# Inverse norm stored ahead of the first tile's load, second weights loaded sooner, ninth mean behind item 3, copies of two means moved

## The chip, the core and the metric

The kernel runs on one core of a Trainium2 chip. A core has five engines, each with a queue of its own: TensorE (PE in the profile; its weight loads are PEld), VectorE (DVE), ScalarE (ACT), GpSimd (POOL) and SyncE (SP, which here only issues DMAs). POOL issues DMAs too: those that add into their target. Both kinds run on the core's 16 DMA engines. Engines wait for each other by semaphores. The metric is the device time of one execution in microseconds (us), lower is better.

## The reference, cut to what matters

```python
X = np.fft.fft(x, axis=1); X = np.fft.fft(X, axis=2)      # x (2, 3008, 256)
x = X.real.reshape(6016, 256)
rms = np.sqrt(np.mean(x * x, axis=-1, keepdims=True) + 1e-06)
xn = x / rms * rms_g
g, val = xn @ w_gate, xn @ w_val                           # 256 -> 1536 each
x = (g / (1.0 + np.exp(-g)) * val) @ w_out                 # 1536 -> 256
h = x @ w_in                                               # 256 -> 2048
out = (h * np.cos(h)) @ w_out2                             # 2048 -> 256
```

## The kernel before, in words

**Stage one, the transform.** The two Fourier transforms are done as matrix products over pairs of tokens that are mirror images (N = 502 pairs make a tile; six tiles, three for each of the two batches). A loop over 34 steps G runs on TensorE: `features(G)`, then `sequence` two or three steps behind. ACT copies two steps' results at a time out of PSUM in `uv_copy(p)`, p = G // 2. The result is u and v, stored to DRAM in pieces (`store_uv`) and loaded again a tile at a time (`load_tile`, `load_u128`).

**The norm.** The rows are cut into nine parts, and each part's mean of squares is numbered 0 to 8 (`MEANS` = 9). For each: ACT squares (`square`, L669), POOL adds the two halves (`add_squares`, L1096), TensorE sums over partitions with one product (`rms`, L504), ACT copies the row out of PSUM adding epsilon (`mean_copy`, L677), and SP spreads it over partitions (`spread_mean`, L334). `RMS_AT` lists the steps G behind which `rms(0)` to `rms(6)` stand, `MEAN_COPY_AT` the steps p of their copies; `rms(7)` and `rms(8)` stand inside the first tile. There are two buffers for the copied row, so copy q waits until the transfer of row q - 2 has landed. Means 0 and 1 are enough for the first tile: ACT takes a root, DVE the reciprocal, POOL a Newton step (`inverse(0)`), SP stores the inverse norm to DRAM (`store_inv`, L343) and loads it back broadcast (`load_inv`, L359), POOL scales uv and u128 (`scale_uv`, `scale_u128`), ACT and DVE split uv into a high and a low part (`split_uv` L717, `lo_part` L906), and TensorE may begin tile 0.

**Stage two, the layers.** A float32 product is made of three: high by high, high by low, low by high (`three`, L518 to L520). A tile has 12 items of the first layer (i = 0 to 11) and 16 of the second. For an item of the first layer: `up1(t, i)` in two halves (gate, then value), DVE adds the 256th feature's part and makes both tokens (`plus_part` L966, `one_token` L974 and L975), ACT the silu (L779), POOL the product (L1158), ACT the high part (`hi1`, L738), DVE and POOL the low part (L951, L1069), and `down(t, i - 2)` follows `up1(t, i)` on TensorE. The stage's order of work on each engine is written out by hand.

**The weights.** They are split in the first tile, between other work. w1 comes in six chunks of 512 KB and wo1 (called `wo1_raw`, the first layer's output weights) in three of 512 KB: ACT writes the high part and the negated high part, and POOL issues a DMA that adds the raw value to it (`w1_add(n)` L1078, `wo1_add(n)` L1084). TensorE waits for `wo1_lo_done[1]` ahead of `down(0, 4)`. wo2 and win2 (2 MB each, the second layer's) are loaded by SP: wo2 behind `spread_mean(8)`, and win2 into the place of w1's raw chunks, so behind the last `w1_add`. ACT, in item 6 of tile 0, waits for `win2_in` and for `wo1_lo_done[2]` (L790, L791) before it splits win2; item 6's `hi1` comes behind that.

SP's queue from the first spread to tile 0's end is one list, in this order: `spread_mean(0)`, first part of `store_uv(0)`, `spread_mean(1)`, `load_tile(0)`, `load_u128(0)`, `store_inv(0)`, `load_inv(0)`, `spread_mean(2)`, rest of `store_uv(0)`, `spread_mean(3)`, wo1, `spread_mean(4)`, `spread_mean(5)` to `(8)`, wo2, `store_uv(1)`, win2.

Of the kernel before, what the change touches and what calls it, by code (L numbers as in the profile page):

```python
# [15 lines left out]
K1 = N1 // 2 + 1  # L16
# [59 lines left out]
def build(nc, x, w1a, w1b, small, wo1, win2, wo2, t_seq1, t_feat, t_seq2, t_const, out):  # L76
    ctx = ExitStack()
    with ctx:
# [149 lines left out]
            b, k = PART_ROWS[q]  # L228
            return b * STEPS + k.stop - 1

        RMS_AT = [8, 9, 15, 21, 24, 28, 32]
        MEAN_COPY_AT = [2, 3, 7, 10, 11, 13, 15]
        RMS_LATE = range(len(RMS_AT), MEANS)

        def rms_bank(q):
            return 3 if q < len(RMS_AT) else 6 + q - len(RMS_AT)

        def parts_ending(p):
            return [q for q in range(MEANS) if part_end(q) // 2 == p]
# [4 lines left out]
        def bank_pair(q):  # L244
            return 2 * (q % 2)
# [11 lines left out]
        W1_SPLIT_AT = {3: 0, 4: 1, 9: 2, 11: 3}  # L257
        W1_NEGATE_AT = {12: 0, 15: 1}
        W1_EARLY = len(W1_NEGATE_AT)
        WO1_SPLIT_AT = {14: 0}  # L260
        W1_SPLIT_LATE, WO1_SPLIT_LATE = {1: 4, 2: 5}, {3: 1, 4: 2}
        LATE_WIN2 = [7, 8]
        WIN2_ORDER = [0, 4, 1, 5, 2, 6, 3, 7]
# [40 lines left out]
        def _(sp):  # L304
            def load(dst, src, s):
                sp.dma_start(dst, src).then_inc(s, 16)  # L306
# [47 lines left out]
            def load_tile(t):  # L354
                sp.dma_start(uv_t[:, :, :], uv_dram[:, :, bass.ds(t * N, N)].rearrange(
                    "u p n -> p u n")).then_inc(uv_in, 16)

            def load_inv(t):
                sp.dma_start(inv_t[:, :], inv_dram[0, bass.ds(t * N, N)].partition_broadcast(P)  # L359
                             ).then_inc(inv_in, 16)  # L360

            def load_u128(t):
                sp.dma_start(u128[:, :], uv_dram[1, 0, bass.ds(t * N, N)].partition_broadcast(P)
                             ).then_inc(u128_in, 16)
# [3 lines left out]
            spread_mean(1)  # L368
            sp.wait_ge(uv_stored, UV_FIRST)
            sp.wait_ge(pq_done, STEPS)  # L370
            load_tile(0)
            load_u128(0)
            sp.wait_ge(inv_done, 1)
            store_inv(0, (slice(0, 1), slice(1, FIRST_ROWS)), 0)
            sp.wait_ge(inv_out, INV_OUT[0])
            load_inv(0)
            spread_mean(2)
            store_uv(0, (slice(FIRST_ROWS, K1 - 1), slice(K1 - 1, K1)))
            spread_mean(3)
            sp.wait_ge(n1_done, 2 * NG)  # L380
            load(wo1_raw[:, :], wo1, wo1_in)
            spread_mean(4)
            sp.wait_ge(uv_stored, UV_BATCH)
            for q in STAT_MEANS[2]:
# [46 lines left out]
        def _(pe):  # L431
# [63 lines left out]
            def rms(q):  # L495

                a, z = part_cols(q)
                pe.wait_ge(const_in, 16)
                pe.wait_ge(sq_added, q + 1)
                if 0 < q < len(RMS_AT):  # L500
                    pe.wait_ge(mean_out, q)
                if q >= len(RMS_AT):
                    pe.wait_ge(uv_main, LAST - 2)
                nc.tensor.matmul(ps[0:1, rms_bank(q), 0:z - a], mean_w, squares[:, q % SQUARES, 0, 0:z - a],  # L504
                                 start=True, stop=True).then_inc(ms_done, 1)

# [67 lines left out]
            def tile(t, first=False):  # L574
                if not first:
                    pe.wait_ge(uv_split, t + 1)
                    up1(t, 0, halves=(0,))
                    down(t - 1, ITEMS - 2)
                    up1(t, 0, halves=(1,))
                up1(t, 1, halves=(0,))  # L580
                if first:
                    rms(RMS_LATE[0])
                else:
                    down(t - 1, ITEMS - 1, tokens=(0,))
                up1(t, 1, halves=(1,))
                if not first:
                    down(t - 1, ITEMS - 1, tokens=(1,))
                for i in range(2, C1):
                    up1(t, i, halves=(0,))
                    if first and i == 2:  # L590
                        rms(RMS_LATE[1])
                    up1(t, i, halves=(1,))
                    if first and i == 2:
                        pe.wait_ge(uv_main, LAST)
                        down(t, 0, tokens=(0,))
                        pe.wait_ge(mean_out, MEANS)
                        down(t, 0, tokens=(1,))
                    else:
                        down(t, i - 2)
                down(t, C1 - 2)  # L600
                down(t, C1 - 1)
                for j in range(C2):
                    up2(t, j)
                    if j >= 2:
                        down(t, C1 + j - 2)
# [15 lines left out]
        def _(act):  # L621
# [97 lines left out]
            for p in range(LAST // 2):  # L719
                if p == 5:  # L720
                    root(0)
                uv_copy(p)
                if p == 13:
                    split_uv(0)
                for q in parts_ending(p):
                    if q < MEANS - 1:
                        square(q)
                for q in means_copied(p):
                    mean_copy(q)
                split_step(p)  # L730


            def hi1(t, i):
# [32 lines left out]
            def tile(t, first=False, last=False):  # L766
                for i in range(C1):
                    if i == 2 and not first:
                        y_copy(t)
                    if first and i == 1:  # L770
                        act.wait_ge(uv_stored, UV_BATCH)
                    if i:
                        hi1(t, i - 1)
                        if first and i == 1:
                            mean_copy(RMS_LATE[1])
                    elif not first:
                        hi2(t - 1, C2 - 1, token_parts(C2 - 1, False))
                    act.wait_ge(g_ready, C1 * t + i + 1)
                    nc.scalar.activation(work[i % 3][:, :, :], work[i % 3][:, :, :], ACT.Silu  # L779
                                         ).then_inc(silu_done, 1)  # L780
                    if first and i == 0:
                        square(MEANS - 1)
                        mean_copy(RMS_LATE[0])
                    if first and i in W1_SPLIT_LATE:
                        split_w1(W1_SPLIT_LATE[i])
                    if first and i in WO1_SPLIT_LATE:
                        split_wo1(WO1_SPLIT_LATE[i])
                    if first and 6 <= i < 10:
                        if i == 6:
                            act.wait_ge(win2_in, 16)  # L790
                            act.wait_ge(wo1_lo_done[WO1_CHUNKS - 1], 16)  # L791
                        win2_part(2 * (i - 6))
                        win2_part(2 * (i - 6) + 1)
                    if first and i == 5:
                        root(1)
                        root(2)
                    if first and C1 - 5 <= i < C1 - 1:
                        k = i - (C1 - 5)
                        if k == 0:
                            act.wait_ge(wo2_in, 16)  # L800
                        wo2_part(k)
# [48 lines left out]
        def _(dve):  # L850
# [87 lines left out]
            for G in range(LAST):  # L938
                pq_copy(G)
                split_step(G)  # L940
                if G == 31:
                    dve.wait_ge(uv_hi_done, 1)
                    lo_part(uv_lo[:, :, 0:N], uv_t[:, :, :], uv_hi[:, :, 0:N], uv_split)
                if G in W1_NEGATE_AT:
                    negate_w1(W1_NEGATE_AT[G])
                if G == 14:
                    recip(0)
# [119 lines left out]
        def _(pool):  # L1067
# [61 lines left out]
            w1_add(1)  # L1129
            add_squares(5)  # L1130
            scale_uv(0)
            add_squares(6)
            w1_add(2)
            scale_u128(0)
            w1_add(3)
            wo1_add(0)
            add_squares(7)

            def wo2_part(k):
                c = slice(k * 512, (k + 1) * 512)  # L1140
# [12 lines left out]
            def tile(t, first=False, last=False):  # L1153
                for i in range(C1 - 1):
                    pool.wait_ge(silu_done, C1 * t + i + 1)
                    pool.wait_ge(v_ready, (C1 - 1) * t + i + 1)
                    for g in product_order(i):
                        nc.gpsimd.tensor_tensor(work[i % 3][:, g, :], work[i % 3][:, g, :],  # L1158
                                                value[i % 2][:, g, :], ALU.mult).then_inc(h_done[g], 1)
                    if first and i == 0:  # L1160
                        add_squares(MEANS - 1)
                    if i == C1 - 2:
                        lo1(t, i, 0, hid_before_last)
                    lo1(t, i, 1, hid_ready_first)
                    if first and i in W1_SPLIT_LATE:
                        w1_add(W1_SPLIT_LATE[i])
                    if first and i in WO1_SPLIT_LATE:
                        wo1_add(WO1_SPLIT_LATE[i])
                    if first and i in LATE_WIN2:
                        win2_part(LATE_WIN2.index(i))  # L1170
# [80 lines left out]
```

## Time and profile before

| what | value |
|---|---|
| median of 3 runs | 987.53 us (987.35 to 987.87) |
| the profiled execution | 989.1 us, its span in the trace 987.1 us |
| TensorE busy | 976.0 us, 99% of the span |
| DVE, ACT, POOL busy | 743.3, 640.9, 349.5 us |
| granted TensorE clock | 1.00 throughout |
| DMA over the span | 36.77 MB |

Busy time is the sum of an engine's instructions in the trace; TensorE's ends are modelled and neighbours overlap. Times in the rows are microseconds from the start of the span. A bracket at the end of a row of the timeline gives how long the engine sat idle ahead of it, and who released it. The time to landing of a DMA counts from the start of its issue.

### The profile page before, as it was taken

The numbers are of one execution on the slowest core, as the hardware profiler recorded it, in microseconds if no ns is written. First come the engines' busy times: TensorE is split into PE (matmuls) and PEld (weight loads), VectorE is DVE, ScalarE is ACT, GpSimd is POOL, SyncE is SP. The second block draws the span as 40 slices with busy tenths as digits, with TensorE's granted clock in tenths as the row PEclk, the third lists the DMA queues.
The fourth block names the chain that finished last, engine by engine and source line by source line (L and its number), as shares of the span: only waits on it lengthen the run. The fifth ranks groups of instructions, "written<-read, shape, count | busy, mean of one in ns | idle before, by whom it ended". The sixth has DMA issues, their size and how long they took to land.

```text
span 987.1 us, 12908 instructions
## 1 busy us (share of the span) xinstructions
PE 976.0 (99%) x4468; PEld 808.4 (82%) x4468; DVE 743.3 (75%) x1028; ACT 640.9 (65%) x801; POOL 349.5 (35%) x292
## 2 busy tenths in 40 slices
PE   8989999999999999999999999999999999999998
PEld 8868788888888888888888888888888888888886
DVE  6779878768877668877768887767887767887665
ACT  5578778774468775358775348776447876437777
POOL 0359776017640007650006751005761003771000
PEclk9999999999999999999999999999999999999999
DMA  9689202001010001010001010001000000100001
GB/s 328 170 202 258 61 1 53 1 1 43 1 42 2 0 1 42 0 32 10 0 0 42 0 32 11 0 0 42 0 29 3 0 0 0 42 0 0 0 0 42
DMA packets 14079, 36.77 MB, mean 37 GB/s; under 512 B 2616, under 2 KB 6680, under 8 KB 13656
## 3 DMA queue, kind: packets, MB, share of 16 engines
q1 hardware_dynamic: 11976, 31.62, 9.4%
q0 software_dynamic: 2064, 4.72, 2.7%
q8 instruction: 14, 0.23, 0.1%
q14 instruction: 25, 0.20, 0.1%
HBM read 22.33 MB, written 9.26 MB: 32 GB/s over the span
## 4 chain that ended last, share of the span: by engine, by line
PE 93%; DMA 2%; POOL 2%; DVE 2%; ACT 1%; issue 0%; SPq 0%; ACTq 0%; DVEq 0%
PE ps L518 30%; PE ps L519 30%; PE ps L520 30%; PE ps L474 2%; POOL work L1158 1%; DMA x_sb<-x 1%; DMA wo_lo<-wo_raw 1%; PE ps L492 1%; PE ps L490 1%; PE ps L504 1%; POOL h_lo L1069 0%; SPq L306 0%; DVE x_sb L857 0%; PE ps L460 0%; DVE uv_lo L906 0%
## 5 line engine op out<-in xcount | busy, mean ns | idle before, releaser
L518 PE MATMUL ps<-h_hi,wo_hi 128*128 128x502 f32 x672 | 261.5, 389 | 0.0
L520 PE MATMUL ps<-h_hi,wo_lo 128*128 128x502 f32 x672 | 261.5, 389 | 0.0
L519 PE MATMUL ps<-h_lo,wo_hi 128*128 128x502 f32 x672 | 261.4, 389 | 0.0
L1069 POOL TENSOR_TENSOR h_lo<-work,h_hi 128x502 fp32r<-128x502 f32 x92 | 101.8, 1114 | 372.9 <-ACT h_hi L753 369.9
L738 ACT ACTIVATE h_hi<-work 128x502 fp32r<-128x502 f32 x132 | 82.6, 626 | 173.9 <-POOL work L1158 173.8
L1056 DVE SCALAR_TENSOR_TENSOR work<-work,ps 128x1004 f32<-128x1004 f32 (+1 forms) x109 | 117.2, 1075 | 95.1 <-ACT work L835 94.7
L1042 DVE SCALAR_TENSOR_TENSOR work<-work,ps 128x1004 f32<-128x1004 f32 (+1 forms) x109 | 116.5, 1074 | 48.6 <-ACT work L821 48.5
L518 PE MATMUL ps<-x_hi,win_hi 128*128 128x502 f32 x384 | 150.0, 391 | 0.0
L519 PE MATMUL ps<-x_lo,win_hi 128*128 128x502 f32 x384 | 149.3, 389 | 0.0
L520 PE MATMUL ps<-x_hi,win_lo 128*128 128x502 f32 x384 | 149.2, 389 | 0.0
L518 PEld LDWEIGHTS ps<-h_hi,wo_hi 128*128 128x128 f32 x672 | 126.3, 188 | 26.7 <-DVE h_lo L959 0.6
L520 PEld LDWEIGHTS ps<-h_hi,wo_lo 128*128 128x128 f32 x672 | 126.3, 188 | 25.9
L519 PEld LDWEIGHTS ps<-h_lo,wo_hi 128*128 128x128 f32 x672 | 126.3, 188 | 25.7
L966 DVE SCALAR_TENSOR_TENSOR plus<-u,w,ps 128x502 f32<-128x502 f32 x144 | 105.8, 735 | 52.4 <-PE ps L520 51.7
L821 ACT ACTIVATE work<-ps 128x1004 f32<-128x1004 f32 (+1 forms) x109 | 98.2, 906 | 60.7 <-PE ps L520 59.9
L830 ACT ACTIVATE work<-work 128x1004 f32<-128x1004 f32 (+1 forms) x109 | 102.8, 943 | 31.1 <-DVE work L1042 30.3
L1158 POOL TENSOR_TENSOR work<-work,uv_t 128x502 f32<-128x502 f32 x72 | 99.1, 1399 | 47.0 <-DVE uv_t L975 45.0
L959 DVE TENSOR_TENSOR h_lo<-work,h_hi 128x502 fp32r<-128x502 f32 x172 | 114.2, 702 | 1.3
L518 PE MATMUL ps<-uv_hi,w_hi 128*128 128x502 f32 x288 | 112.7, 391 | 2.3 <-ACT mean_row L677 1.4
L520 PE MATMUL ps<-uv_hi,w_lo 128*128 128x502 f32 x288 | 111.9, 389 | 0.0
L519 PE MATMUL ps<-uv_lo,w_hi 128*128 128x502 f32 x288 | 111.9, 389 | 0.0
L753 ACT ACTIVATE h_hi<-work 128x1004 fp32r<-128x1004 f32 (+1 forms) x109 | 101.7, 938 | 14.6 <-PE ps L520 8.7
(87 smaller groups left out, 1282.0 us busy)
## 6 DMA issues: line engine op xcount, KB each, us to landing
out<-y_sb SPq DMA_DIRECT2D x10, 502.0 KB, 3.2
x_sb<-x SPq DMA_DIRECT2D x6, 768.0 KB, 10.8
w_lo<-w_f POOLq DMA_DIRECT2D x6, 512.0 KB, 7.6
uv_t<-uv_dram SPq DMA_DIRECT2D x6, 502.0 KB, 3.6
wo_raw<-wo SPq DMA_DIRECT2D x1, 2048.0 KB, 8.8
win_raw<-win SPq DMA_DIRECT2D x1, 2048.0 KB, 10.0
raw_b<-w1b SPq DMA_DIRECT2D x3, 512.0 KB, 12.8
raw_a<-w1a SPq DMA_DIRECT2D x3, 512.0 KB, 13.1
```

The lines of the kernel that those rows point to most:

```text
L518: nc.tensor.matmul(acc, w_hi, v_hi, start=start, stop=False)
L519: nc.tensor.matmul(acc, w_hi, v_lo, start=False, stop=False)
L520: return nc.tensor.matmul(acc, w_lo, v_hi, start=False, stop=stop)
L753: nc.scalar.activation(h_hi[j % 2][:, gs, 0:N], work[j % 4][:, gs, :], ACT.Copy).then_inc(hi_done, gs.stop - gs.start)
L821: nc.scalar.activation(work[j % 4][:, gs, :], ps[:, bank_pair(j) + gs.start:bank_pair(j) + gs.stop, 0:N], ACT.Copy, bias=MAGIC).then_inc(r ...
L830: nc.scalar.activation(work[j % 4][:, gs, :], work[j % 4][:, gs, :], ACT.Sin, scale=TURN / 2).then_inc(sin_done, gs.stop - gs.start)
L959: nc.vector.tensor_tensor(h_lo[j % 2][:, g, 0:N], work[j % 4][:, g, :], h_hi[j % 2][:, g, 0:N].bitcast(F32), ALU.subtract).then_inc(hid_sp ...
L966: nc.vector.scalar_tensor_tensor(out=plus[m][:, :], in0=u128[:, :], scalar=w128[:, m * C1 + i:m * C1 + i + 1], in1=ps[:, bank_pair(m), 0:N ...
L1042: nc.vector.scalar_tensor_tensor(out=buf, in0=buf, scalar=MAGIC, in1=pair, op0=ALU.subtract, op1=ALU.subtract).then_inc(frac_done, gs.stop ...
L1056: nc.vector.scalar_tensor_tensor(out=buf, in0=buf, scalar=1.0, in1=pair, op0=ALU.subtract, op1=ALU.mult).then_inc(cos_done, gs.stop - gs.s ...
L1069: nc.gpsimd.tensor_tensor(dst, src, hi.bitcast(F32), ALU.subtract).then_inc(s, 1)
L1158: nc.gpsimd.tensor_tensor(work[i % 3][:, g, :], work[i % 3][:, g, :], value[i % 2][:, g, :], ALU.mult).then_inc(h_done[g], 1)
```

## The change

It has five parts. **SP's queue:** `store_inv(0)` ahead of `load_tile(0)`; `load_u128(0)` behind `load_inv(0)`; wo1's load ahead of `spread_mean(3)` and of the rest of `store_uv(0)`. **Two means moved:** `rms(3)` behind step 20 instead of 21, its copy at p = 9 instead of 10. **The ninth mean:** `rms(8)` moves from between the halves of `up1(0, 2)` to behind `down(0, 1)` in item 3, writes bank 2, and TensorE waits for its copy between the halves of `up1(0, 4)`; ACT's copy moves from item 1, ahead of its silu, to the end of item 3, behind `split_wo1(1)`; POOL's `add_squares(8)` goes behind the low part of item 0. **First tile's split:** `split_uv(0)` at p = 12 (was 13), `lo_part` at G = 30 (was 31), `split_wo1(0)` at p = 15 (was 14), with a Silu on one element behind the last uv copy. **POOL's queue:** `scale_u128(0)` and `w1_add(2)` ahead of `add_squares(6)`, `add_squares(7)` ahead of `wo1_add(0)`.

```diff
-        RMS_AT = [8, 9, 15, 21, 24, 28, 32]
-        MEAN_COPY_AT = [2, 3, 7, 10, 11, 13, 15]
+        RMS_AT = [8, 9, 15, 20, 24, 28, 32]
+        MEAN_COPY_AT = [2, 3, 7, 9, 11, 13, 15]
+        LAST_MEAN_AT = 3
         def rms_bank(q):
-            return 3 if q < len(RMS_AT) else 6 + q - len(RMS_AT)
+            return 3 if q < len(RMS_AT) else 6 if q < MEANS - 1 else bank_pair(1)
-        WO1_SPLIT_AT = {14: 0}
+        WO1_SPLIT_AT = {15: 0}
@@ sync
-            load_tile(0)
-            load_u128(0)
             sp.wait_ge(inv_done, 1)
             store_inv(0, (slice(0, 1), slice(1, FIRST_ROWS)), 0)
+            load_tile(0)
             sp.wait_ge(inv_out, INV_OUT[0])
             load_inv(0)
+            load_u128(0)
             spread_mean(2)
-            store_uv(0, (slice(FIRST_ROWS, K1 - 1), slice(K1 - 1, K1)))
-            spread_mean(3)
             sp.wait_ge(n1_done, 2 * NG)
             load(wo1_raw[:, :], wo1, wo1_in)
+            spread_mean(3)
+            store_uv(0, (slice(FIRST_ROWS, K1 - 1), slice(K1 - 1, K1)))
             spread_mean(4)
@@ tensor, rms(q)
-                if q >= len(RMS_AT):
+                if q == RMS_LATE[0]:
                     pe.wait_ge(uv_main, LAST - 2)
+                if q == RMS_LATE[1]:
+                    pe.wait_ge(plus_done, 2 * LAST_MEAN_AT + 2)
@@ tensor, tile
                     up1(t, i, halves=(0,))
-                    if first and i == 2:
-                        rms(RMS_LATE[1])
+                    if first and i == LAST_MEAN_AT + 1:
+                        pe.wait_ge(mean_out, MEANS)
                     up1(t, i, halves=(1,))
                     if first and i == 2:
                         pe.wait_ge(uv_main, LAST)
                         down(t, 0, tokens=(0,))
-                        pe.wait_ge(mean_out, MEANS)
+                        pe.wait_ge(mean_out, MEANS - 1)
                         down(t, 0, tokens=(1,))
                     else:
                         down(t, i - 2)
+                    if first and i == LAST_MEAN_AT:
+                        rms(RMS_LATE[1])
@@ scalar
-                if p == 13:
+                if p == 12:
                     split_uv(0)
+            act.wait_ge(recip_done, 1)
+            nc.scalar.activation(stat[0:1, 1, 0:1], stat[0:1, 1, 0:1], ACT.Silu)
@@ scalar, tile
-                        if first and i == 1:
-                            mean_copy(RMS_LATE[1])
                     if first and i in WO1_SPLIT_LATE:
                         split_wo1(WO1_SPLIT_LATE[i])
+                    if first and i == LAST_MEAN_AT:
+                        mean_copy(RMS_LATE[1])
@@ vector
-                if G == 31:
+                if G == 30:
                     dve.wait_ge(uv_hi_done, 1)
                     lo_part(uv_lo[:, :, 0:N], uv_t[:, :, :], uv_hi[:, :, 0:N], uv_split)
@@ gpsimd
             scale_uv(0)
+            scale_u128(0)
+            w1_add(2)
             add_squares(6)
-            w1_add(2)
-            scale_u128(0)
             w1_add(3)
+            add_squares(7)
             wo1_add(0)
-            add_squares(7)
@@ gpsimd, tile
-                    if first and i == 0:
-                        add_squares(MEANS - 1)
                     if i == C1 - 2:
                         lo1(t, i, 0, hid_before_last)
                     lo1(t, i, 1, hid_ready_first)
+                    if first and i == 0:
+                        add_squares(MEANS - 1)
```

## Rows read from the trace of the kernel before

**Rows 1.** The page: busy time of each engine, share of the span, instructions

```profile
PE 976.0 (99%) x4468; PEld 808.4 (82%) x4468; DVE 743.3 (75%) x1028; ACT 640.9 (65%) x801; POOL 349.5 (35%) x292
```

**Rows 2.** Timeline of TensorE: start, duration, line, operation, tiles, count, idle before it

```profile
51.68 0.64 PE L504 MATMUL ps<-squares,consts 128*1 128x282 f32 x2 [1.09 <-ACT mean_row L677]
...
62.63 0.47 PE L518 MATMUL ps<-uv_hi,w_hi 128*128 128x502 f32 x1 [0.57 <-DVE uv_lo L906]
...
66.44 0.49 PE L518 MATMUL ps<-uv_hi,w_hi 128*128 128x502 f32 x1 [1.35 <-ACT mean_row L677]
...
73.95 0.95 PE L504 MATMUL ps<-squares,consts 128*1 128x470 f32 x2 [0.79 <-issue]
...
85.82 0.39 PE L518 MATMUL ps<-uv_hi,w_hi 128*128 128x502 f32 x1
...
98.06 0.39 PE L518 MATMUL ps<-h_hi,wo_hi 128*128 128x502 f32 x1
...
114.48 0.49 PE L518 MATMUL ps<-uv_hi,w_hi 128*128 128x502 f32 x1 [0.37 <-DVE uv_t L975]
```

**Rows 3.** Chain that ended last, 94 us on: start, duration, what

```profile
94.11 11.20 DMA wo_lo<-wo_raw
```

**Rows 4.** Timeline of ACT

```profile
74.94 0.55 ACT L677 ACTIVATE mean_row<-ps 1x470 f32<-1x470 f32 x1 [1.40 <-PE ps L504]
...
86.41 1.06 ACT L702 ACTIVATE wo_lo<-wo_hi 128x1024 fp32r<-128x1024 f32 x1
...
105.39 1.16 ACT L707 ACTIVATE win_hi<-win_raw 128x512 fp32r<-128x512 f32 x2 [3.83 <-DMA wo_lo<-wo_raw]
```

**Rows 5.** Timeline of SP's queue: DMA issues, merged where they follow each other

```profile
44.26 0.84 SPq L343 DMA_DIRECT2D inv_dram<-stat  x2
...
54.59 21.64 SPq L334 DMA_DIRECT2D stat<-mean_row  x5
76.27 0.43 SPq L306 DMA_DIRECT2D wo_raw<-wo  x1
76.75 1.76 SPq L351 DMA_DIRECT2D uv_dram<-uv  x3
94.06 0.35 SPq L306 DMA_DIRECT2D win_raw<-win  x1
```

**Rows 6.** Timeline of POOL

```profile
57.80 0.85 POOL L1096 TENSOR_TENSOR squares<-squares 128x376 f32<-128x376 f32 x1 [1.20 <-ACT squares L669]
...
80.08 1.21 POOL L1078 DMA_DIRECT2D w_lo<-w_f  x1
80.86 2.98 POOL L1158 TENSOR_TENSOR work<-work,uv_t 128x502 f32<-128x502 f32 x2
...
89.30 1.15 POOL L1084 DMA_DIRECT2D wo_lo<-wo_raw  x1
```

**Rows 7.** Timeline of DVE

```profile
68.11 0.74 DVE L966 SCALAR_TENSOR_TENSOR plus<-u,w,ps 128x502 f32<-128x502 f32 x1 [1.74 <-PE ps L520]
...
80.04 0.67 DVE L975 TENSOR_TENSOR uv_t<-plus,ps 128x502 f32<-128x502 f32 x1
```

**Rows 8.** Stretches: engines' busy us and count, clock, DMA share, GB/s

```profile
76.00:77.00 1.00, 1.00 (x7) 0.81 (x6) 1.00 (x3) 1.00 (x2) 0.50 (x1) 1.00 0.01 2
77.00:78.00 1.00, 1.00 (x6) 0.84 (x5) 0.97 (x2) 0.97 (x2) 1.00 (x2) 1.00 1.25 246
...
80.00:82.00 2.00, 2.00 (x11) 1.66 (x10) 1.95 (x4) 1.97 (x3) 2.00 (x3) 1.00 1.02 410
...
104.00:106.00 2.00, 2.00 (x11) 1.65 (x10) 1.90 (x4) 0.61 (x2) 0.14 (x1) 1.00 0.03 6
```

**Rows 9.** DMA issues at 80.08, 89.30 and 94.06: size, us to landing

```profile
w_lo<-w_f POOLq DMA_DIRECT2D x1, 512.0 KB, 11.1
...
wo_lo<-wo_raw POOLq DMA_DIRECT2D x1, 512.0 KB, 7.1
...
win_raw<-win SPq DMA_DIRECT2D x1, 2048.0 KB, 10.0
```

More of the change, by code:

```diff
@@ L229, in part_end @@
             return b * STEPS + k.stop - 1
-        RMS_AT = [8, 9, 15, 21, 24, 28, 32]
-        MEAN_COPY_AT = [2, 3, 7, 10, 11, 13, 15]
+        RMS_AT = [8, 9, 15, 20, 24, 28, 32]
+        MEAN_COPY_AT = [2, 3, 7, 9, 11, 13, 15]
         RMS_LATE = range(len(RMS_AT), MEANS)
+        LAST_MEAN_AT = 3
+        assert len(RMS_LATE) == 2
         def rms_bank(q):
-            return 3 if q < len(RMS_AT) else 6 + q - len(RMS_AT)
+            return 3 if q < len(RMS_AT) else 6 if q < MEANS - 1 else bank_pair(1)
         def parts_ending(p):
```

## The prediction

> **What bounds the kernel now.** I read the page's busy times first: TensorE is busy 99% of the span, the next engine 75% [rows 1], at full clock. So an edit can gain only what TensorE waits, and I listed its idle time in its timeline. Behind the transform's start there are five waits: 1.09 us for a mean's copy at 51.68, 0.57 for the low part of uv at 62.63, 1.35 for the seventh mean's copy at 66.44, 0.79 ahead of the ninth mean's product at 73.95, and 0.37 at 114.48 [rows 2]. Sum 4.17 us, 0.42% of the span: the ceiling for this change.
>
> The last one is small but is the tip of a chain, and that chain decides. Read backward: TensorE at 114.48 waits for DVE's value tokens of item 8. DVE came late because it had waited for ACT's high part of item 6, and ACT had stood 3.83 us, until 105.39, for the last wo1 add [rows 4]. The chain of waits gives that add as one piece of DMA, 94.11 to 105.3 [rows 3], for 512 KB. It stood in a queue. Then I read the stretches by DMA share: nothing at 76 to 77, full from 77, nothing again from 104 [rows 8]. What started it is in SP's timeline: five spreads merged until 76.23, and right behind them wo2 at 76.27, the three stores of batch 1 by 78.5, win2 at 94.06 [rows 5]. wo2 is queued behind `spread_mean(8)`, and that waits for the ninth mean's copy, which ended at 75.49 [rows 4]. From 77.2 to 105.3, 28.1 us, the DMA engines work off wo2, uv, four adds and win2, and ACT needs the last of them. There is no slack between this backlog's end and TensorE: it already costs 0.37.
>
> **The parts, one by one.**
>
> *SP's queue, the two means moved, the first split sooner.* No work is added; two more issues of SP stand ahead of `load_tile(0)` (0.84 us [rows 5]) and cost nothing, since `store_inv` no longer stands behind the tile's loads and the inverse norm is back sooner. `rms(3)` and its copy one step sooner take away the 1.09 wait. Uv is split one step sooner on ACT and DVE, which takes the 0.57. `split_wo1(0)` waited for wo1 ahead of the seventh mean's copy; behind it, the 1.35 goes. What is late next: TensorE now reaches `rms(6)` 1.09 sooner, and POOL's addition for it ran at 57.80 as soon as ACT's square was there [rows 6]. In the new order the split of uv stands ahead of that square on ACT, and the copy ahead of `rms(6)` needs the transfer of mean 3, now queued behind wo1's 1.5 MB. I let 0.7 of the 1.09 come back there. TensorE so reaches the value half of item 0 (66.44 before) 0.4 + 0.57 + 1.35 = 2.3 us sooner, at 64.1. Bounds: 0 if mean 4's transfer, now behind wo1 and the uv stores, delays the seventh copy as much as wo1 did; 3.0 if all three waits go. The one-element Silu brings a table load forward that ACT does anyway. The reorder on POOL moves `scale_u128` and one add by about a microsecond, with POOL idle 1.20 there [rows 6]: nothing.
>
> *`rms(8)` leaves item 2.* The wait of 0.79 and the 0.95 of the product go from there. I give it nothing: DVE is busy without a pause from its first wait at 68.11 to past 80 and ends the value tokens of item 2 at 80.71 [rows 7], when TensorE was 0.4 from needing them, so TensorE only waits for DVE instead. POOL's product of item 2 began at 80.86, on those tokens [rows 6]; ACT's silu and what follows hang on it. So ACT keeps its distance to TensorE's start: 2.3 sooner, no more.
>
> *`rms(8)` in item 3.* The product costs its 0.95 there. Its copy stands on ACT behind `split_wo1(1)`, whose second instruction ended at 86.41 + 1.06 = 87.47 [rows 4]. With 0.5 for the copy and 2.3 off: it ends at 85.7, while it ended at 75.49. TensorE needs it ahead of the value half of item 4, which began at 85.82 before [rows 2]. The 2.3 us are used up by the product and a wait of a good 1 us; at item 4 TensorE stands where it stood before. This far the change is worth -0.1 to -0.3.
>
> *What is queued behind that copy.* `spread_mean(8)`, and behind it wo2, the three stores and win2: 10.2 us later, wo2 at 86.5 instead of 76.27. In exchange w1's last two adds, issued at 80.08 and four us later, meet an idle DMA and leave the backlog. What one is worth: the add issued at 80.08 landed 11.1 later, at 91.2, the next let win2 be issued at 94.06, the one issued at 89.30 landed 7.1 later, at 96.4 [rows 5, 6, 9]: 2.9 and 2.3, so 2.6 each, 5.3 for both. The backlog is then 28.1 - 5.3 = 22.8 us and begins 10.2 later: it ends at 77.2 + 10.2 + 22.8 = 110.2, not 105.3. ACT starts win2's split 4.9 later, and as the chain to 114.48 has no slack, TensorE's wait there grows by 4.9 plus the little it is early. All behind it moves along.
>
> The Trainium skill's page on DMA (DMA: Bandwidth & Descriptors, Specifications) gives the fabric a ceiling of 435 GB/s. By that the plain transfers would take 13.2 us, an estimate, the backlog 18.5, and the change would come out near 0.5 us slower; the best stretch here reaches 410 [rows 8], the whole backlog much less.
>
> **The sum.** Against the execution's own span of 987.1 (its time 989.1): +4.9, a span of 992.0. The median of the runs shown is 987.53, and I add the same: 992.4 us, +0.5%.
>
> **The rivals.**
>
> 1. *The wo1 add for item 4 starves.* TensorE needs `wo1_add(1)` at 98.06 [rows 2]. It is issued some 2 us behind the late copy, behind wo2 and the stores, about 1 us ahead of win2. In order of arrival it lands near 101.3: TensorE stands 3 us, hidden under the later wait, as from 98.06 to the wait before 114.48 are 16.0 us of products [rows 2] and that half is free at 119.4. Later than 103.4 it shows. If win2 goes first, it lands near 108 and the change costs about 9.5 us: 997.0. For it: win2 took 10.0 to land [rows 9] with an add beside it landing after. Against: the add issued at 80.08 waited its 11.1 behind what had come first [rows 6, 9], which is order of arrival. Chance 0.17.
>
> 2. *The first part gains little.* If the seventh copy waits for mean 4's transfer, the 2.3 shrinks to 0 to 1, and all of it is added: +6 to +7.2, 994. Chance 0.13.
>
> 3. *The backlog is absorbed.* The other side, by one mechanism: with fewer adding DMAs mixed in, plain transfers run at the 410 GB/s of the stretch at 80 [rows 8]. The plain transfers' 5.74 MB (wo2 and win2 2.10 each, the stores 1.54: 3 tiles of 502 pairs, two numbers, 128 partitions, 4 bytes) take 14.0, two adds 5.3: 19.3 us, end at 106.7. Then +1.4: 988.9. Faster than that, from an end before 105, TensorE's last wait goes too: 987.0. It decides at a backlog of 17.9 us. Against it: 28.1 less four adds leaves 17.5 for the same bytes, 328 GB/s. Chance 0.1.
>
> 4. *Faster.* The copy of mean 8 comes as soon as its product, because ACT is early enough to have the split done; then wo2 is only some 7 us late, the backlog ends by 107, and if the transfers also run faster the early waits remain won: 987.5 less up to 3 of the 4.2 waits, 985. It needs POOL's product of item 2 some 3 us sooner, and the tokens at 80.71 [rows 7] forbid that. Chance 0.05.
>
> **The numbers.** My forecast, +3.5 to +6.2, has 0.55; the likeliest one's own range is 991.0 to 993.7. The range of 8 in 10 goes from rival 3's upper part to rival 1: 989.8 to 997.2. What a measurement of this kernel can tell from no change is about 0.2%, 2 us. Slower: 0.55 + 0.17 + 0.13 = 0.85. Same: rival 3, 0.1. Faster: 0.05.
>
> **What the profile would show.** TensorE's waits near 51.68, 62.63 and 66.44 gone, one new of 0.3 to 1.2 before `rms(6)`; the value half of item 0 near 64. No wait in item 2 for a mean, but short ones for DVE. The ninth copy ending near 85.7, and a wait of about 1 us before item 4's value half. SP's wo2 near 86.5, the DMA share near nothing from 82 to 87 and full to about 110; a wait on wo1's add near 98; ACT's wait for the last add about 8 us long, and in TensorE waits from 98 to 120 that sum to 5. Behind 120 nothing new. The prediction is wrong if the ninth copy ends before 80, if the DMA backlog is done before 107, or if ACT is not what TensorE waits for there.

## The result, and the profile after

Five runs of each kernel: 996.62 us median after (995.27 to 1000.3), 987.87 before (987.35 to 992.09). The ratio is 1.0084 with a 95% interval of 1.0058 to 1.0109, or +8.3 us, +5.7 to +10.8. The profiled execution took 996.14 us with a span of 994.0, against 989.1 and 987.1 before: in the traces the loss is 6.9 us. The profiled execution of before happened to lie 1.2 above its median and that of after 0.5 below, which is nearly all of the difference between 6.9 and 8.75.

What made that execution of before longer can be seen. Its wait of 1.35 us at 66.44 [rows 2] came from ACT, which stood 2.22 us for wo1's load ahead of `split_wo1(0)`. Five of the runs below (3, 4, 5, 9 and 11) have the same code up to there. ACT stood 0.61 to 0.88 us in four of them and TensorE had no wait at this place; in run 11 it was 1.43 and 0.55. From the gate half of item 0 to its value half it is 3.81 us in before, 3.02 in run 11 and 2.23 to 2.27 in the other four. ACT in before, then ACT and TensorE in run 9:

```profile
63.52 1.06 ACT L700 ACTIVATE wo_hi<-wo_raw 128x1024 fp32r<-128x1024 f32 x1 [2.22 <-DMA wo_raw<-wo]
```

```profile
61.28 1.06 ACT L701 ACTIVATE wo_hi<-wo_raw 128x1024 fp32r<-128x1024 f32 x1 [0.61 <-DMA wo_raw<-wo]
```

```profile
62.19 0.47 PE L519 MATMUL ps<-uv_hi,w_hi 128*128 128x502 f32 x1 [0.77 <-DVE uv_lo L907]
...
64.42 0.47 PE L519 MATMUL ps<-uv_hi,w_hi 128*128 128x502 f32 x1
```

So some 1.5 us of what the change seems to win at item 0 belong to a wait that most of these traces do not have.

TensorE's timeline after, at the rows that answer to [rows 2]:

```profile
59.27 0.79 PE L508 MATMUL ps<-squares,consts 128*1 128x376 f32 x2 [0.84 <-POOL squares L1104]
...
63.57 0.47 PE L522 MATMUL ps<-uv_hi,w_hi 128*128 128x502 f32 x1
...
76.59 0.50 PE L522 MATMUL ps<-uv_hi,w_hi 128*128 128x502 f32 x1 [0.95 <-DVE plus L974]
...
86.95 0.49 PE L522 MATMUL ps<-uv_hi,w_hi 128*128 128x502 f32 x1 [0.92 <-ACT mean_row L683]
...
99.29 0.39 PE L522 MATMUL ps<-h_hi,wo_hi 128*128 128x502 f32 x1
...
114.46 0.79 PE L522 MATMUL ps<-h_hi,wo_hi 128*128 128x502 f32 x1 [4.13 <-DVE h_lo L959]
...
119.40 0.39 PE L522 MATMUL ps<-uv_hi,w_hi 128*128 128x502 f32 x1
```

Read it as a race of one kernel against the other, at the same product each time. The value half of item 0 begins at 63.57, 2.87 us ahead of the profiled execution of before. The value half of item 4 begins at 86.95, 1.13 behind [rows 2]: four us are gone in between. `down(0, 4)` at 99.29 is 1.23 behind. `down(0, 6)` at 114.46 is 5.52 behind (108.94 before), after a wait of 4.13. The wait that before has one product group later, at 114.48, has moved up to this place. Item 9 begins at 119.40, 7.74 behind (111.66 before). Before then loses 0.9 in its own last waits, and the spans end 6.9 apart. The two rows of the kernel before that this uses:

```profile
108.94 0.39 PE L518 MATMUL ps<-h_hi,wo_hi 128*128 128x502 f32 x1
...
111.66 0.39 PE L518 MATMUL ps<-uv_hi,w_hi 128*128 128x502 f32 x1
```

SP's queue and ACT, which answer to [rows 5] and [rows 4]:

```profile
52.81 34.83 SPq L336 DMA_DIRECT2D stat<-mean_row  x5
87.68 0.43 SPq L308 DMA_DIRECT2D wo_raw<-wo  x1
88.16 1.89 SPq L353 DMA_DIRECT2D uv_dram<-uv  x3
90.30 0.35 SPq L308 DMA_DIRECT2D win_raw<-win  x1
```

```profile
86.36 0.54 ACT L683 ACTIVATE mean_row<-ps 1x470 f32<-1x470 f32 x1
...
111.05 1.15 ACT L713 ACTIVATE win_hi<-win_raw 128x512 fp32r<-128x512 f32 x2 [8.27 <-DMA win_raw<-win]
```

The five spreads now hold SP until 87.64, and wo2 is issued at 87.68, 11.4 later than before. ACT stands 8.27 us in item 6, until 111.05, 5.7 later. What releases it is win2, and not the last wo1 add as before: that add, issued at 94.65, landed 10.8 us later, at 105.4, and win2 took from 90.30 to 111.0:

```profile
win_raw<-win SPq DMA_DIRECT2D x1, 2048.0 KB, 20.7
```

The stretches (engines' busy us and count, clock, DMA share, GB/s) show both ends of the backlog and something behind it:

```profile
82.00:84.00 2.00, 2.00 (x9) 1.05 (x8) 1.90 (x4) 1.45 (x3) 2.00 (x3) 1.00 0.00 0
...
86.00:88.00 2.00, 1.08 (x6) 0.91 (x6) 1.83 (x3) 1.88 (x4) 2.00 (x3) 1.00 1.12 193
...
108.00:110.00 2.00, 2.00 (x11) 1.59 (x9) 0.00 (x0) 0.00 (x0) 0.00 (x0) 1.00 0.44 188
110.00:112.00 2.00, 0.33 (x2) 0.00 (x0) 0.00 (x0) 0.95 (x2) 0.00 (x0) 1.00 0.02 8
112.00:114.00 2.00, 0.00 (x0) 0.00 (x0) 0.74 (x1) 2.00 (x4) 1.08 (x1) 0.57 0.02 4
114.00:116.00 2.00, 1.54 (x4) 1.28 (x5) 1.91 (x4) 2.00 (x4) 1.77 (x2) 0.50 0.00 0
...
120.00:122.00 2.00, 2.00 (x11) 1.65 (x10) 1.62 (x4) 1.23 (x3) 1.76 (x2) 1.00 0.00 0
```

The DMA engines do nothing at 82 to 84, where before they were in the middle of the backlog:

```profile
82.00:84.00 2.00, 2.00 (x10) 1.66 (x9) 1.92 (x3) 1.46 (x3) 2.00 (x3) 1.00 0.88 264
```

And while TensorE stood, its granted clock fell from 1.00 to 0.50, that is from 2.4 to 1.2 GHz, and stayed there until about 119. `down(0, 6)`, twelve products, took 4.94 us (114.46 to 119.40) instead of 2.72: 2.2 us that no wait shows.

What made the ninth copy late, on DVE and POOL:

```profile
72.46 1.75 DVE L935 SCALAR_TENSOR_TENSOR w_f<-raw_a,sm,raw_b 128x512 f32<-128x512 f32 x1
74.14 1.75 DVE L935 SCALAR_TENSOR_TENSOR w_f<-raw_a,gvec,raw_b 128x512 f32<-128x512 f32 x1
```

```profile
71.96 3.38 POOL L1166 TENSOR_TENSOR work<-work,work 128x502 f32<-128x502 f32 x2
```

The two late mixes of w1 (in which DVE makes the weights of a chunk out of the raw ones) took 1.75 us each; before it was 0.74 each, when POOL's product of item 1 began only behind them and took 2.62:

```profile
75.34 0.74 DVE L927 SCALAR_TENSOR_TENSOR w_f<-raw_a,sm,raw_b 128x512 f32<-128x512 f32 x1
76.00 0.74 DVE L927 SCALAR_TENSOR_TENSOR w_f<-raw_a,gvec,raw_b 128x512 f32<-128x512 f32 x1
```

```profile
76.50 2.62 POOL L1158 TENSOR_TENSOR work<-work,work 128x502 f32<-128x502 f32 x2 [1.62 <-ACT work L779]
```

Run 3 (the ninth mean's part alone) has 1.75, 1.75 and 3.39, run 2 (without that part) 0.74, 0.74 and 2.62. In the changed kernel nothing holds ACT for the ninth mean in item 1, so POOL's product begins early and lies over both mixes. That makes DVE 2 us later for item 2's tokens, and TensorE, silu, product and the ninth copy follow.

### The profile page after: what moved, and what is told of

It reads as the page before. It is cut to its first block, busy times and chain, and to the rows that moved or that the text cites. A ratio compares the mean times of both kernels' runs of the same rounds, so it can differ in the third digit from the quotient of the medians.

```text
span 994.0 us, 12909 instructions
## 1 busy us (share of the span) xinstructions
PE 978.7 (98%) x4468; PEld 809.1 (81%) x4468; DVE 743.0 (75%) x1028; ACT 640.8 (64%) x802; POOL 351.4 (35%) x292
## 4 chain that ended last, share of the span: by engine, by line
PE 91%; DMA 3%; DVE 2%; POOL 2%; issue 1%; SPq 1%; ACT 0%; DVEq 0%; POOLq 0%; ACTq 0%
PE ps L522 30%; PE ps L523 29%; PE ps L524 29%; DMA win_raw<-win 2%; DMA x_sb<-x 1%; PE ps L476 1%; PE ps L494 0%; POOL work L1166 0%; PE ps L492 0%; SPq L308 0%; DVE plus L974 0%; DVE w_f L935 0%; POOL uv_t L1123 0%; POOL w_lo L1086 0%; POOL squares L1104 0%
## 6 DMA issues: line engine op xcount, KB each, us to landing
x_sb<-x SPq DMA_DIRECT2D x6, 768.0 KB, 10.5
```

## The experiments

Each median stands against runs of the kernel before that were taken beside it on the same chip. Differences in us are that ratio less one, times 988, and two experiments are compared by their ratios.

**1. The queue freed: wo2 ahead of the ninth spread, in the changed kernel.**

```diff
-            for q in STAT_MEANS[2]:
+            for q in STAT_MEANS[2][:-1]:
                 spread_mean(q)
             sp.wait_ge(uv_done, LAST)
             load(wo2_raw[:, :], wo2, wo2_in)
             store_uv(1, (slice(0, 1), slice(1, K1 - 1), slice(K1 - 1, K1)))
+            spread_mean(MEANS - 1)
```

> The changed kernel with one edit on SP's queue: wo2's load and the three stores of batch 1 stand ahead of spread_mean(8) instead of behind it. Everything else of the change stays, the late ninth copy too. Theory A (the time goes to what is queued behind the ninth copy on SP): the DMA backlog starts near 70 us and is done before 103, ACT waits less than 1 us for the last add, the wait of 4.1 us and the half clock behind it vanish; TensorE is 1.1 late at item 4 and gets back the 0.4 to 0.9 of the old last wait: 987.5 to 989. Theory B (the ninth product and its copy in item 3 cost by themselves, on TensorE, ACT and DVE): no more than 2 us come back, 994 to 996.

Measured: 989.97, ratio 1.0017 (1.0009 to 1.0026), clock 1.00. The wait of 4.13 and the half clock are gone, so 6.6 of 8.3 us came back by one transfer moved on SP, and theory B (no more than 2) is out. +1.7 is left, and the median is 1 us above theory A's range: here the ninth copy still ends at 87.0, and win2 is issued at 88.98.

```profile
69.30 0.44 SPq L308 DMA_DIRECT2D wo_raw<-wo  x1
69.79 1.69 SPq L353 DMA_DIRECT2D uv_dram<-uv  x3
87.01 0.73 SPq L336 DMA_DIRECT2D stat<-mean_row  x1
88.98 0.36 SPq L308 DMA_DIRECT2D win_raw<-win  x1
```

**2. The change without the ninth mean's part.** All edits of `rms(8)`, its copy, its bank and its addition undone; the others kept:

```diff
-                    if first and i == LAST_MEAN_AT:
-                        rms(RMS_LATE[1])
...
+                    if first and i == 2:
+                        rms(RMS_LATE[1])
...
+                        if first and i == 1:
+                            mean_copy(RMS_LATE[1])
```

> The changed kernel without the ninth mean's part: rms(8), its copy, its bank and its addition stand where they stood before; SP's queue, the two moved means, the earlier split of uv and POOL's reorder stay. Theory A: wo2 is issued near 73.5 us and the backlog ends near 102; what the first parts won at item 0 (2.9 us in the changed kernel's trace) is kept: 984.5 to 986. Rival (the first parts' gain is lost again in items 1 to 3 because DVE sets the pace there): 987 to 988. Theory C (the first parts themselves make the time longer by wo1 ahead of the stores): above 990.

Measured: 986.5, ratio 0.9981 (0.9973 to 0.9990): -1.9 us, where theory A had -2 to -3.5; the direction is clear of noise, the median is 0.5 above its range. That range started from the 2.9 us of the traces at item 0, of which some 1.5 belong to that wait of 1.35. Of five waits, TensorE keeps two by more than 0.5: 0.84 ahead of `rms(6)` and 0.80 ahead of `rms(8)` in item 2. wo2 goes out at 73.74.

**3. The ninth mean's part alone, in the kernel before.** The same edits put into the kernel before, nothing else.

> The kernel before with only the ninth mean's part of the change. Theory A: item 0 starts where it did before, so the ninth copy ends near 89, wo2 is issued near 90, ACT is released near 113.5, and TensorE's wait and its clock behind it cost 9 to 12 us: 997 to 1000. Theory C (the first parts cause the loss): 987.5 to 989.

Measured: 997.74, ratio 1.0099 (1.0081 to 1.0116): +9.8 us, as theory A had it. This part loses alone what the whole change loses, and about 1.5 more, and theory C is out; 2 and 3 together (-1.9 and +9.8) give +7.9, and the change measured +8.3. ACT's rows:

```profile
87.56 0.54 ACT L683 ACTIVATE mean_row<-ps 1x470 f32<-1x470 f32 x1
...
112.06 1.15 ACT L713 ACTIVATE win_hi<-win_raw 128x512 fp32r<-128x512 f32 x2 [8.07 <-DMA win_raw<-win]
```

**4. Only wo2 late, in the kernel before.**

```diff
             sp.wait_ge(uv_done, LAST)
+            sp.wait_ge(plus_done, 9)
             load(wo2_raw[:, :], wo2, wo2_in)
```

> The kernel before with one added wait on SP: wo2's load waits for DVE's gate half of item 4 (near 86.9 us), which is where the changed kernel issues it. No mean is moved, no other edit. Theory A: ACT is released near 110.5, TensorE stands some 5 us and then runs at half clock for a few us: +5.5 to +9, 993.5 to 997, so nearly the whole loss of the change with none of its parts. Theory B: 987.5 to 989.

Measured: 997.04, ratio 1.0082 (1.0065 to 1.0099): +8.1 us, the upper end of theory A; wo2 goes out at 86.30. No mean is touched, no product is moved, and the change's whole loss is there. TensorE:

```profile
98.75 0.49 PE L519 MATMUL ps<-h_hi,wo_hi 128*128 128x502 f32 x1 [1.07 <-DMA wo_lo<-wo_raw]
...
114.50 0.79 PE L519 MATMUL ps<-h_hi,wo_hi 128*128 128x502 f32 x1 [4.61 <-DVE h_lo L952]
```

Here the second wo1 add is also 1.07 late for `down(0, 4)`, the first rival's mechanism in small.

**5. Half the dose.** `sp.wait_ge(plus_done, 7)` in the same place; in its trace wo2 goes out at 80.54.

> The kernel before with wo2's load waiting for DVE's gate half of item 3 (near 82 us) instead of item 4. Half the dose of the run before it. wo2 5.8 us later than 76.27, and one of w1's two adds (2.6 us) leaves the backlog: ACT is released near 108.5, 3.2 later, and TensorE waits some 3.2 us ahead of down(6). Theory A, with the clock: if a wait of 3 us also drops the clock as the waits of 4 us did, 992.5 to 994; if the clock stays at its upper level, 990.5 to 991.5. Theory B (when wo2 is loaded does not matter): 988.

Measured: 992.02, ratio 1.0043 (1.0029 to 1.0056): +4.2 us. The traces differ by 2.7 (span 989.8). That is less than the medians' 4.2 because this trace has no wait at item 0, where before has its 1.35. The median lies between the two forms that were expected. In the profiled execution the clock stayed at 1.00, and of the six executions the three at 1.00 took 991.3 to 991.7 and the three with a mean clock of 0.998 took 992.3 to 993.0. So the plain wait gives most of it, and the clock adds to it in some executions. The size was short also because a second wait of 1.04 us, for the wo1 add, came with it.

```profile
97.78 0.49 PE L519 MATMUL ps<-h_hi,wo_hi 128*128 128x502 f32 x1 [1.04 <-DMA wo_lo<-wo_raw]
...
111.36 0.49 PE L519 MATMUL ps<-h_hi,wo_hi 128*128 128x502 f32 x1 [2.43 <-DVE h_lo L952]
```

The first product after the wait takes 0.49 us here and 0.79 in the run before it: that is where the clock shows first.

**6. The two mixes of w1 taken out of item 1**, with wo2 ahead as in 1:

```diff
-        MIX_AT = [3, 5, 8, 9, 16, 18, 20, 22, 24, 26]
-        MIX_LATE = [10, 11]
+        MIX_AT = [3, 5, 8, 9, 16, 18, 20, 22, 24, 26, 31, 32]
+        MIX_LATE = []
```

> The changed kernel with wo2 ahead of spread_mean(8), and also DVE's last two mixes of w1 moved from item 1 of the first tile to steps 31 and 32 of the transform, where DVE stood 1.6 us. In the changed kernel these two took 1.75 us each instead of 0.74, beside POOL's product. Theory D (the collision in item 1 makes DVE late, and that costs the waits of 0.95, 0.34 and 0.39 us in item 3 and puts the ninth copy off by some 2 us): those waits go or shrink below 0.3, the ninth copy ends near 84.5, 1.7 to 3 us less than the same kernel with the mixes in item 1: 986.5 to 988.3. Rival (DVE is not what items 2 and 3 wait for, or the mixes delay the transform): no less than 989.5.

Measured: 987.62, ratio 0.9994 (0.9982 to 1.0005): 2.3 us less than 1, as theory D had it. TensorE's wait of 0.95 in item 3 and those of 0.34 and 0.39 are gone, that for the ninth copy is down to 0.20 and the copy ends at 85.15. It is not free: the first mix waits 2.19 us on DVE for w1's second add, and TensorE stands 0.73 at 62.8.

**7. The ninth copy ahead of `split_wo1(1)` as well.**

```diff
+                    if first and i == LAST_MEAN_AT:
+                        mean_copy(RMS_LATE[1])
                     if first and i in WO1_SPLIT_LATE:
                         split_wo1(WO1_SPLIT_LATE[i])
-                    if first and i == LAST_MEAN_AT:
-                        mean_copy(RMS_LATE[1])
```

> The same as the mixes early, and also ACT's copy of the ninth mean ahead of split_wo1(1) instead of behind it in item 3. Theory: TensorE's wait of 0.93 us between the halves of item 4 goes, and nothing else waits for split_wo1(1) that early, so about 0.9 us less than the run before it: 985.5 to 987.5. Rival: with the mixes early the copy is no longer waited for, or POOL's wo1 add comes later by the copy and its landing delays down(0, 4): same as the run before it.

Measured: 988.49, ratio 1.0007 (0.9998 to 1.0015), no better than 6. A miss: the wait for the copy went, but TensorE stands 1.02 us at 97.88 for the second wo1 add. The rival that named this add had it. The add was issued at 87.31 and win2 at 87.30, and it took 10.5 us to land; in run 6, with win2 1.9 us behind it, it took 5.0.

**8. The first parts with wo2 ahead of the ninth spread**, and **9. the kernel before with only that.** The edit is that of 1.

> The changed kernel with the ninth mean as before and wo2 with the three stores ahead of spread_mean(8): both halves of what the runs so far showed. Theory A: the backlog begins near 70 us and is done before 99, ACT's wait for the last add (4.1 us in the run with the ninth mean as before) goes, and with it the last 0.4 to 0.9 us of TensorE's waits: 985.3 to 986.2, some 0.5 us less than that run and the best of all. Rival (the last wait is set by DVE's own queue, or the stores issued sooner slow the mean's transfer): the same as that run, 986.5.

> The kernel before with only wo2 and the three stores of batch 1 ahead of spread_mean(8). Theory A says that the kernel before already paid 0.4 to 0.9 us at 114.48 for this order: 987.0 to 987.6, the last wait gone from the trace, the other four unchanged. Rival: no difference, because the transfers of w1's last adds come later in the queue and hold win2 as before: 987.9, the wait still there.

Measured: 988.37, ratio 0.9997 (0.9983 to 1.0011), and 990.37, ratio 1.0022 (1.0011 to 1.0033). Both medians are worse than those of the same kernel with wo2 left where it was (986.5 and 988.1), against theory A and its rival. For run 9 this is clear of noise. Run 8's executions spread from 985.22 to 989.93: three are as fast as run 2's, five took 989.8 with a mean clock of 0.998, and the two ratios' intervals overlap, so its loss of 1.6 us is less certain. wo2 sooner is not simply better. TensorE and SP in 8:

```profile
97.46 0.49 PE L519 MATMUL ps<-h_hi,wo_hi 128*128 128x502 f32 x1 [2.29 <-DMA wo_lo<-wo_raw]
```

```profile
72.47 0.73 SPq L334 DMA_DIRECT2D stat<-mean_row  x1
86.87 0.36 SPq L306 DMA_DIRECT2D win_raw<-win  x1
```

POOL issued the second wo1 add at 86.26, SP win2 at 86.87, and the DMA issues of that stretch with their us to landing were:

```profile
win_raw<-win SPq DMA_DIRECT2D x1, 2048.0 KB, 9.6
wo_lo<-wo_raw POOLq DMA_DIRECT2D x1, 512.0 KB, 11.2
```

Four times the bytes, issued 0.6 us later, landed 1 us sooner (96.5 against 97.5). With wo2 where it was, w1's last adds stand behind it, win2 waits for them on SP until 91.65, and the wo1 add goes first. If this race is the cause, the old order held win2 back by accident. The next two runs test it.

**10 and 11. The same two with win2 behind the landing of the second wo1 add.**

```diff
             for n in range(W1_CHUNKS):
                 sp.wait_ge(w1_lo_done[n], 16)
+            sp.wait_ge(wo1_lo_done[1], 16)
             load(win2_raw[:, :], win2, win2_in)
```

> The run with the first parts and wo2 ahead, and one wait more on SP: win2's load waits until wo1's second add has landed. In the two runs with wo2 ahead and an unblocked SP, TensorE stood 2.3 and 2.6 us ahead of down(0, 4) near 97 for that add: win2 (2 MB) was issued within 1 us of it. Theory E (win2 in front of the add is the whole of it): the wait at 97 goes, the add lands near 92, win2 is issued near 92 and lands near 100, ACT waits 1 to 3 us in item 6, which TensorE does not feel or feels by 0.4: span 983.5 to 984.8, median 985.3 to 986.5, at or below the run with the ninth mean as before. Rival (the loss comes from the stores or wo2 earlier beside the transform's end): the median stays at 988.

> The kernel before with wo2 and the stores ahead of spread_mean(8) and win2's load behind the landing of wo1's second add. Theory E: the 2.6 us wait at 98 of the run without the second edit goes, TensorE's last wait of 0.4 too: 987 to 988, so 2.4 us less than that run. Rival: 990.

Measured: 986.6, ratio 0.9983 (0.9973 to 0.9992), and 987.97, ratio 0.9999 (0.9990 to 1.0008). The waits at 97 and 98 are gone in both, 1.4 and 2.3 us less than 8 and 9 by their ratios: theory E. In run 10 the second wo1 add, issued at 86.31, landed 4.8 us later, where in run 8 it took 11.2:

```profile
wo_lo<-wo_raw POOLq DMA_DIRECT2D x1, 512.0 KB, 4.8
```

Run 10 is as fast as run 2, not faster; the two ratios' intervals lie on each other. Run 2 or 10 is the best of the study, 1.7 to 1.9 us under the kernel before. Theory E had two sizes wrong. ACT waits 4.12 us in 10 for the last add, where it had 1 to 3. And TensorE's last wait of before, 0.37 at 114.48, is still there, 0.39 in both, though it should have gone in 11.

## Why the prediction was right, and where it was off

It forecast slower, 992.4 within 989.8 to 997.2; the measured median is 996.62. The mechanism is the one given, and the size was short: +8.75 by the medians for +4.9. The likeliest range of its own, 991.0 to 993.7, was missed. The wide range reached to 997.2 for the sake of rival 1, which did not happen, so that 996.62 lies inside it is in part luck.

- **What bounds the kernel.** Right: the wait at 114.48 was the end of a chain from the ninth copy through SP's queue and the DMA backlog. Run 4 shows it with nothing else changed.
- **SP's queue, moved means, earlier split.** Forecast 2.3 sooner at item 0, measured 2.87 against the profiled execution of before, but 1.2 against run 3, which has the old code there. The 1.35 was counted as a gain, and it is a wait that four of five other traces of that code do not have. The wait that comes back ahead of `rms(6)` is 0.84, where 0.7 was put. What this part gives to the time was not separated in the forecast; run 2 gives -1.9.
- **`rms(8)` out of item 2.** "I give it nothing" was right in its reason (TensorE waits for DVE instead: 0.32, 0.46, then 0.95) and missed that it costs. POOL's product then falls on DVE's two mixes. Run 6 took them out of the way and got 2.3 us.
- **The ninth copy.** Forecast to end at 85.7, measured 86.90; the 2 us of the collision, less the 0.6 that item 0 began sooner than forecast, are most of the difference. TensorE's wait ahead of item 4's value half: "a good 1 us", measured 0.92.
- **The backlog.** wo2 at 87.68 instead of 86.5; ACT released at 111.05 instead of 110.2. From wo2's issue to the release it is 29.1 us before and 23.4 after, so w1's two adds were worth 5.7, not 5.3, if all of the difference is put down to them. This step, the main term, measured +5.7 for a forecast of +4.9, and the DMA engines were idle only to about 85 and not to 87. The last transfer to land was win2 and not the last add.
- **The term that was missing.** The sum let TensorE wait and then go on at full speed. Its clock halved, which cost 2.2 us more. Of the old waits behind, 0.9 was given back. So 5.5 + 2.2 - 0.9 = 6.8 of the 6.9 in the trace.
- **The trace's difference set on the median.** The forecast added its +4.9 to the median, but had taken it from an execution 1.2 us above it, with the 1.35 among the gains. That is 1.2 of the 1.7 us by which the medians differ more than the traces.
- **Rival 1**, the wo1 add that starves, did not decide, nor did the wait near 98 that the main forecast had: the add issued at 88.50 landed 10.3 later, at 98.8 and not at 101.3, and TensorE began at 99.29 without a wait. It was 0.5 us away, and in runs 4, 5, 7, 8 and 9 it is there with 1 to 2.6 us. In 4 and 5 the add took 9.9 us, no longer than here, and TensorE came for it at 97.7 and 96.7; in 7, 8 and 9 win2 went out within 0.7 us of the add.
- **Rival 3**, a backlog that runs faster with fewer adds in it: not so. It would have needed a backlog of 17.9 us from the first byte. From wo2's issue, which before was some 1 us ahead of the first byte, it took 23.4.
- **Rivals 2 and 4** did not happen: the seventh copy was not late (no wait at item 0), and the ninth copy ended at 86.90, not early.

The other 0.5 us of the 1.7 stays open. Runs of the changed kernel show mean clocks of 0.996 to 0.998, so the clock's part differs from run to run, but only one trace of it was looked at.

## What to carry to other kernels

When an operation is moved, follow what is queued behind it on every engine that waits for it, DMA queues first: the ninth mean's copy cost nothing in itself, but 5.7 MB of weights and results stood behind its spread. A transfer that must be early should not stand in one queue behind a wait that it does not need, and where two transfers race, the order should be written as a wait and not left to a backlog. A wait of some us on TensorE should be priced with the products behind it, at the clock that the rows show there. And where the profiled execution lies above the median, its waits are not all gains to be had: a wait that comes and goes from one execution to the next should be left out of the sum, or looked up in a second trace.

## What the runs showed of the hardware

- The granted clock fell to 0.50 behind a TensorE wait of 4.13 us in the changed kernel, 3.91 in run 3 and 4.61 in run 4. It stayed at 1.00 behind 2.43 in run 5 and 2.29 in run 8, in their profiled executions; three of six and five of twelve executions of these two have a mean clock of 0.998, and no trace shows where it fell there. In run 9, behind 2.62, it fell too, for some 3 us:

```profile
98.00:100.00 2.00, 1.23 (x3) 1.06 (x4) 1.56 (x3) 1.47 (x2) 0.44 (x1) 0.65 1.03 205
100.00:102.00 2.00, 2.00 (x6) 1.57 (x6) 0.00 (x0) 0.65 (x2) 2.00 (x2) 0.50 0.08 18
```

  At the lower level six products fit into the 2 us of its second stretch, where eleven fit elsewhere, and in the changed kernel `down(0, 6)` took 4.94 us instead of 2.72.
- A DVE mix of two SBUF operands took 1.75 us beside POOL's product and 0.74 without, and two of POOL's products took 3.38 instead of 2.62. By the Trainium skill (SBUF — State Buffer, section SBUF: two separate sides) a DVE operation with two SBUF inputs and a GpSimd operation that reads SBUF share one pair of ports, which the one that starts first holds for its whole instruction. The trace agrees that both get longer.
- Two transfers on different queues did not share evenly. In run 8 the 2 MB of win2, issued 0.6 us behind a 512 KB add, landed 1 us ahead of it. The Trainium skill (DMA: Bandwidth & Descriptors, section Queues, rings and completion order) has each DMA engine go round its queues packet by packet. In this trace that does not protect the smaller transfer: from 86 to 98 the packets of SP's queue held 14.6 KB on average and those of POOL's 3.4 KB, so turns by packet would not be equal shares of bytes. From 88 to 92, 72 packets of the one moved and 16 of the other, which is no even alternation either, if both had work waiting. Whether the rule gives the landing is not shown.
- In the changed kernel w1's second add, issued at 47.37 ahead of wo1's load at 47.94, landed 13.8 us later; before, with wo1's load at 53.30, it took 5.5. Nobody waited for it until run 6 moved the mixes.
